# Attention and two mixtures of experts on one core: the projections of the middle stage regrouped, three of them moved to the end of the period ahead, and a new order of all steps

## The chip, the cores and the metric

One NeuronCore of a Trainium2 chip runs the whole program. The metric is the device time of one execution in microseconds (us), lower is better; the number compared is the median over runs.

## The reference

Three layers follow each other on a batch of B = 4 sequences of S = 576 positions, D = 512 columns, all in float32.

```python
# 1: attention, 8 heads of 64: heads 0-3 see the last 32 positions, heads 4-7 every 4th of the last 128
scores = where(mask, (q @ k.T) / 8, -1e9);  x = softmax(scores) @ v            # (B, S, 8*64)
# 2: mixture of 4 causal attention experts, the 2 best of each position
for e in range(4):
    q, k, v = x @ wq[e], x @ wk[e], x @ wv[e]                                  # (B, S, 64)
    ye = softmax(where(causal, -1e9, (q @ k.T) / 8)) @ v @ wo[e]
    out += (gate weight of e at this position) * ye                             # gate: softmax of the 2 best of x @ w_gate
# 3: mixture of 8 feed-forward experts (512 -> 1024 -> 512), one expert a position
e[s] = argmax(logits[s])  if s == 0 or local_gate[s] < 0.5  else e[s - 1]
y[s] = softmax(logits[s])[e] * (relu(out[s] @ w1[e]) @ w2[e])
```

## The kernel before, in words

**Periods.** The first two layers are pipelined over the batch. There are five periods. In period a, TensorE (PE), VectorE (DVE) and ScalarE (ACT) work on layer 1 of sequence a and, at the same time, on layer 2 of sequence m = a - 1. In the first period there is no layer 2 work (m is None), in the last no layer 1 work (a is None). After the five periods DVE and PE work out the routing of layer 3 (`dve_route`, L1599), and the feed-forward experts run slot by slot. The order of the steps in a period is written out by hand, three times: `pe_period` (L801), `act_period` (L1217) and `dve_period` (L1474). Each engine takes its list strictly in order; semaphores tie them together.

**Layer 1 in a period.** Sixteen steps `pe_use` 0 to 15 (L601) transpose queries and keys that the DMAs brought into `raw`, four steps for each of four pairs of heads, through the one PSUM bank `X`; `move_use_d` and `move_use_a` (L1064, L1074) copy them to `qT` and `kT`. Then come 14 groups G of three blocks: `pe_scores` (L620), `dve_mask` (L1371), `act_exp` (L1187), `dve_norm` (L1389), `pe_probs` (L639, the transposes of the probabilities), `move_probs` (L1084), `pe_values` (L652), and `move_x_d`/`move_x_a` (L1107, L1116), which write the result to `XT` or, for the first two pairs of heads, to `xa`. GpSimd (POOL) copies `xa` into `XT` once the projections of the sequence before are done. `pe_values` of group G + 1 waits for the moves of group G, since there is one bank for it.

**Layer 2 in a period.** Thirteen projections `pe_project` 0 to 12 (L673): 0 to 4 are the values with the gate logits (one 128-row tile each, the last 64 rows), 5 to 12 the queries and keys. They go in turn to the two banks `S2`, and `move_proj` (L1137) empties them, even ones on DVE, odd ones on ACT. `dve_gates` (L1401, four parts, with `act_gates` on ACT between) turns the gate logits into `gate`. Then ten units w = 0 to 9: `pe_scores2` (L699), `dve_mask2` and `act_exp2` for each of two heads, `dve_sums2`, `dve_norm2` (which reads `gate`), `pe_probs2` (L724, two halves), `move_probs2`, `pe_values2` (L737), `move_out2`. Two units make one tile of `pe_out` (L755), whose result `move_y` copies out of bank `X` and SP stores. `pe_logits` (L767) makes the router logits of layer 3, `dve_logits` copies them.

**Where a period has nothing to do.** With m None or a None, some steps are skipped and some are replaced by `turn_over` (L615): two products of the identity with itself that nobody reads. `pe_project` and `pe_scores2` do that in the first period, `pe_scores` from group 6 and `pe_values` from group 5 in the last.

**The DMA queue of SP** takes in order, in each period: `load_qk` (L301) of pairs 2 and 3, `load_v` (L312) and the loads for the next period, and `store_y` 0 to 4 (L338); each waits for the step that frees its buffer. Weights, and queries and keys of pair 2 of the first sequence, are issued before the first period.

The period's order on PE before begins and ends so:

```python
pe_project(pe, m, 0); pe_project(pe, m, 1); pe_use(pe, m, a, 0, 0); pe_project(pe, m, 2); ...
... pe_probs2(pe, m, 8, 1); pe_values2(pe, m, 8); pe_probs2(pe, m, 9, 0); pe_probs2(pe, m, 9, 1)
pe_values2(pe, m, 9); pe_logits(pe, m, a); pe_out(pe, m, a, 4, 16)
```

Of the kernel before, what the change touches and what calls it, by code (L numbers as in the profile page):

```python
# [16 lines left out]
P = 128  # L17
# [27 lines left out]
NT = len(TILE)  # L45
# [26 lines left out]
def build(nc, q, k, v, w_gate, wq, wk, wv, wo, w_gate2, w_local, w1, w2, out, xs):  # L72
    with ExitStack() as ctx:
# [276 lines left out]
        def _(sp):  # L350
# [16 lines left out]
            for a in range(B + 1):  # L367
# [304 lines left out]

        def pe_project(pe, m, n):  # L673
            if m is None:
                turn_over(pe, S2[0], 2)
                return
            kind, x, half = proj_piece(n)
            if n == 0:
# [3 lines left out]
                pe.wait_ge(w_loaded, W_LOADS)  # L682
                pe.wait_ge(wor_m, 4)
                if m > 0:
                    pe.wait_ge(masked2, m * SUBS)
            if n >= 2:
                pe.wait_ge(proj_moved[n % 2], m * NPROJ_B[n % 2] + n // 2)
            for c in range(NC):
                if kind == "v":
                    for r in range(0, P, TILE[x]):  # L690
                        last = pe.matmul(S2[n % 2][r:r + TILE[x], 0:VW], XT[:, c, T0[x]:T0[x] + TILE[x]],  # L691
                                         wv_sb[:, c, :], start=(c == 0), stop=(c == NC - 1))
                else:
                    w = wq_sb if kind == "q" else wk_sb
                    last = pe.matmul(S2[n % 2][:, 0:PCOLS], w[:, c, x * P:(x + 1) * P],  # L695
# [3 lines left out]
        def pe_scores2(pe, m, w):  # L699
# [24 lines left out]
        def pe_probs2(pe, m, w, h):  # L724
# [4 lines left out]
            pe.wait_ge(normed2, m * SUBS + c + 1)  # L729
            if m * 2 * UNITS + 2 * w + h > 0:  # L730
# [6 lines left out]
        def pe_values2(pe, m, w):  # L737
# [3 lines left out]
            nq = TILE[t]  # L741
            pe.wait_ge(pt2_moved, m * 2 * UNITS + 2 * w + 2)
# [58 lines left out]
        def pe_period(pe, m, a):  # L801

            pe_project(pe, m, 0)
            pe_project(pe, m, 1)
            pe_use(pe, m, a, 0, 0)
            pe_project(pe, m, 2)
            pe_use(pe, m, a, 1, 0)
            pe_project(pe, m, 3)
            pe_use(pe, m, a, 2, 0)
            pe_project(pe, m, 4)  # L810
            pe_use(pe, m, a, 3, 0)
            pe_project(pe, m, 5)
            pe_scores(pe, a, 0)
            pe_use(pe, m, a, 4, 0)
            pe_project(pe, m, 6)
            pe_scores(pe, a, 1)
            pe_router_turn(pe, m)
            pe_use(pe, m, a, 5, 0)
            pe_probs(pe, a, 0)
            pe_project(pe, m, 7)  # L820
            pe_values(pe, a, 0)
            pe_use(pe, m, a, 6, 0)
            pe_scores(pe, a, 2)
            pe_probs(pe, a, 1)
            pe_project(pe, m, 8)
            pe_use(pe, m, a, 7, 0)
            pe_values(pe, a, 1)
            pe_project(pe, m, 9)
            pe_scores(pe, a, 3)
            pe_probs(pe, a, 2)  # L830
            pe_use(pe, m, a, 8, 0)
            pe_project(pe, m, 10)
            pe_values(pe, a, 2)
            pe_router(pe, m)
            pe_use(pe, m, a, 9, 0)
            pe_scores(pe, a, 4)
            pe_probs(pe, a, 3)
            pe_project(pe, m, 11)
            pe_use(pe, m, a, 10, 0)
            pe_values(pe, a, 3)  # L840
            pe_scores(pe, a, 5)
            pe_probs(pe, a, 4)
            pe_project(pe, m, 12)
            pe_use(pe, m, a, 11, 0)
            pe_values(pe, a, 4)
            pe_scores2(pe, m, 0)
            pe_scores(pe, a, 6)
            pe_probs(pe, a, 5)
            pe_use(pe, m, a, 12, 0)
            pe_scores2(pe, m, 1)  # L850
            pe_values(pe, a, 5)
            pe_scores(pe, a, 7)
            pe_use(pe, m, a, 13, 0)
            pe_probs2(pe, m, 0, 0)
            pe_probs2(pe, m, 0, 1)
            pe_probs(pe, a, 6)
            pe_scores2(pe, m, 2)
            pe_values2(pe, m, 0)
            pe_use(pe, m, a, 14, 0)
# [965 lines left out]
```

## Time and profile before

| | us |
|---|---|
| median of 3 runs (844.21 to 846.16) | 845.7 |
| the profiled execution's own time | 846.1 |
| its span, first to last instruction | 844.4 |
| PE busy | 772.6 (91%) |
| DVE busy | 322.3 (38%) |
| ACT busy | 266.5 (32%) |
| mean granted TensorE clock | 0.952 of full speed |

The five periods fill the span from 0 to 445.4 us; the routing and the feed-forward experts the rest. Busy time of PE counts a matmul for as long as it takes, also where the granted clock is at half, so an idle time and a slow clock have to be looked for separately.

### The profile page before, as it was taken

What the parts mean: (1) busy time and instruction counts of PE and PEld (TensorE: products, weight loads), DVE (VectorE), ACT (ScalarE), POOL (GpSimd) and SP (SyncE); (2) the same over time, 40 slices, a digit from 0 to 9 for tenths busy, and PEclk for the clock granted to TensorE, in tenths of its full rate; (3) what the DMA queues carried; (4) which work ended last, traced back from release to release, by engine and by line L of the source; (5) the groups of instructions that cost most, each with busy time, mean ns of one, the idle gap of its engine ahead of it and who ended that gap; (6) DMA issues with size and microseconds to landing.
All of it is one profiled execution on the core that took longest, in us unless ns stands there. A gap on an engine that the chain in (4) does not pass through costs nothing. (4 is left out here: it accounts for less than half of the span.)

```text
span 844.4 us, 12479 instructions
## 1 busy us (share of the span) xinstructions
PE 772.6 (91%) x3835; PEld 490.0 (58%) x3836; DVE 322.3 (38%) x976; ACT 266.5 (32%) x864; POOL 82.5 (10%) x141
## 2 busy tenths in 40 slices
PE   8879989899989999899987999999999999999980
PEld 8767866578656876576553544545445454444540
DVE  3663587256861588323525611112111121121110
ACT  2662677247761578402430020111101111011000
POOL 4110010000100000000001111101001011010111
PEclk8998999899997999889986999999999999999996
DMA  6852253113620222000003211551151551010010
GB/s 148 167 148 71 56 142 98 39 32 78 177 60 16 58 69 101 26 7 1 28 24 125 98 45 39 224 218 37 37 212 50 223 225 38 25 50 19 26 49 7
DMA packets 88815, 69.62 MB, mean 82 GB/s; under 512 B 78334, under 2 KB 78366, under 8 KB 86848
## 3 DMA queue, kind: packets, MB, share of 16 engines
q1 hardware_dynamic: 81120, 44.73, 18.5%
q0 software_dynamic: 7648, 24.29, 8.7%
q8 instruction: 26, 0.43, 0.2%
q14 instruction: 21, 0.17, 0.1%
HBM read 118.12 MB, written 11.27 MB: 153 GB/s over the span
## 5 line engine op out<-in xcount | busy, mean ns | idle before, releaser
L988 PE MATMUL bank<-w_sb,pt 128*128 x352 | 158.4, 593 | 1.3 <-DVE pt L1765 1.3
L1008 PE MATMUL bank<-w_all,raw_all 128*128 x352 | 154.8, 592 | 2.3 <-DVE raw_all L1769 2.3
L1353 ACT ACTIVATE raw_all<-bank 128x512 f32<-128x512 f32 x44 | 26.3, 597 | 270.3 <-PE bank L988 270.3
L1008 PEld LDWEIGHTS bank<-w_all,raw_all 128*128 128x128 f32 x352 | 65.4, 191 | 76.2 <-issue 76.2
L988 PEld LDWEIGHTS bank<-w_sb,pt 128*128 128x128 f32 x352 | 64.0, 192 | 65.2 <-issue 65.2
L1778 DVE TENSOR_SCALAR raw_all<-bank,p_slot 128x512 f32 x22 | 16.5, 751 | 156.6 <-PE bank L1008 149.4
L695 PE MATMUL bank<-stage_b,w_all 128*128 128x288 f32 x256 | 66.9, 409 | 0.0
L1196 ACT ACTIVATE pr<-sm,negmax_a 96x80 f32<-96x80 f32 (+1 forms) x168 | 59.7, 358 | 8.8 <-DVE negmax_a L1387 8.6
L570 POOL DMA_INDIRECT out_dram<-raw_all,idx x25 | 25.4, 1017 | 288.9 <-DVE raw_all L1778 274.5
L695 PEld LDWEIGHTS bank<-stage_b,w_all 128*128 128x128 f32 x256 | 46.7, 190 | 11.2 <-issue 0.4
L1185 ACT COPY w_sb<-bank 128x256 f32<-128x256 f32 (+3 forms) x81 | 34.6, 427 | 44.5 <-PE bank L733 43.9
L1769 DVE COPY raw_all<-bank 128x512 f32<-128x512 f32 x44 | 30.2, 686 | 46.7 <-PE bank L997 46.7
L1765 DVE COPY pt<-bank 128x512 f32<-128x512 f32 x23 | 15.9, 692 | 82.4 <-PE bank L974 82.4
L763 PE MATMUL bank<-w_all,OT 128*128 128x512 f32 (+1 forms) x80 | 45.5, 697 | 0.0
L635 PE MATMUL bank<-kT,qT 128*96 128x80 f32 (+1 forms) x336 | 43.5, 267 | 1.9 <-DVE negmax_a L1387 1.1
L733 PE MATMUL bank<-ident,heads_out 128*128 128x128 f32 (+1 forms) x200 | 37.0, 283 | 9.0 <-ACT w_sb L1185 8.4
L751 PE MATMUL bank<-w_sb,V 128*64 128x128 f32 (+2 forms) x480 | 33.3, 273 | 11.5 <-ACT w_sb L1185 11.3
L635 PEld LDWEIGHTS bank<-kT,qT 128*96 128x96 f32 (+1 forms) x336 | 38.8, 181 | 5.8 <-DVE negmax_a L1387 2.3
L691 PE MATMUL bank<-w_all,stage_b 128*128 128x260 f32 (+1 forms) x192 | 40.4, 402 | 0.5 <-DVE stage_b L1114 0.5
L733 PEld LDWEIGHTS bank<-ident,heads_out 128*128 128x128 f32 (+1 forms) x200 | 22.8, 142 | 30.2 <-issue 23.0
L997 PEld LDWEIGHTS bank<-ident,raw_all 128*128 128x128 f32 x176 | 27.8, 204 | 19.8 <-issue 19.8
L751 PEld LDWEIGHTS bank<-w_sb,V 128*64 128x64 f32 (+1 forms) x480 | 23.7, 143 | 21.5 <-ACT w_sb L1185 19.5
(212 smaller groups left out, 1029.6 us busy)
## 6 DMA issues: line engine op xcount, KB each, us to landing
w_sb<-in_moe_w_dram SPq DMA_DIRECT2D x19, 2048.0 KB
w_all<-in_moe_w_dram SPq DMA_DIRECT2D x19, 2048.0 KB
w_sb<-in_moe_w_dram POOLq DMA_DIRECT2D x12, 512.0 KB, 4.2
w_all<-in_moe_w_dram POOLq DMA_DIRECT2D x12, 512.0 KB, 4.1
raw_all<-in_q_dram SPq DMA_DIRECT2D x32, 144.0 KB
raw_all<-in_k_dram SPq DMA_DIRECT2D x32, 144.0 KB
mixture_rows<-y_sb SPq DMA_DIRECT2D x16, 256.0 KB, 2.0
v_dil<-in_v_dram SPq DMA_DIRECT2D x48, 80.0 KB, 2.6
```

What stands on the lines that cost most here:

```text
L635: last = pe.matmul(SA[0:M, m * nk:(m + 1) * nk], qT[s][:, blk * M:(blk + 1) * M], kT[s][:, k0:k0 + nk], start=True, stop=True)
L691: last = pe.matmul(S2[n % 2][r:r + TILE[x], 0:VW], XT[:, c, T0[x]:T0[x] + TILE[x]], wv_sb[:, c, :], start=(c == 0), stop=(c == NC - 1))
L695: last = pe.matmul(S2[n % 2][:, 0:PCOLS], w[:, c, x * P:(x + 1) * P], XT[:, c, half * PCOLS:(half + 1) * PCOLS], start=(c == 0), stop=(c = ...
L733: last = pe.transpose(PT[0:TILE[kb], n * P:(n + 1) * P], pr2[c % 2][:, T0[kb]:T0[kb] + TILE[kb]], ident[:, :])
L751: last = pe.matmul(O2[h * DH:(h + 1) * DH, 0:nq], V[0:nk, kb, e * DH:(e + 1) * DH], ptm[0:nk, w % 2, c0:c0 + nq], start=(kb == 0), stop=(k ...
L763: last = pe.matmul(X[0:nq, :], OT[:, p, T0[t]:T0[t] + nq], wo_sb[:, p, :], start=(p == 0), stop=(p == PAIR_E - 1))
L988: last = pe.matmul(ps[half], xT[:, c * P:(c + 1) * P], w1_sb[:, bass.ds(buf, 1), c * F + half * HALF:c * F + (half + 1) * HALF].rearrange( ...
L997: last = pe.transpose(ps[2 + half][:, c * P:(c + 1) * P], hid[:, half * HALF:(half + 1) * HALF].rearrange("x (m c) -> x c m", c=4)[:, c, : ...
L1008: last = pe.matmul(ps[5], hidT[:, n * P:(n + 1) * P], w2_sb[:, bass.ds(buf, 1), n // 4, (n % 4) * D:(n % 4 + 1) * D].rearrange("p o n -> p ...
L1185: return nc.scalar.copy(o, i)
L1196: last = nc.scalar.activation(pr4[G % 4][0:M, m * nk:(m + 1) * nk], sm4[G % 4][0:M, m * nk:(m + 1) * nk], ACT.Exp, bias=negmax[G % 4][0:M, ...
L1769: nc.vector.tensor_copy(hidT[:, half * HALF:(half + 1) * HALF], ps[2 + half]).then_inc(hT_moved[half], 1)
```

## The change: what it does

Five things. (1) The pieces are renumbered: 0 to 7 are now queries and keys, 8 to 12 values with gate logits. (2) The value pieces go to the banks `PT` and `O2` (those of `pe_probs2` and `pe_values2`), by the new `proj_bank`, so `S2` is free for `pe_scores2` once the eight others are moved; its wait is cut to those, and the waits for the rest go to `pe_probs2`, `pe_values2` and `dve_gates`. (3) `pe_project(pe, a, 0)`, `1` and `2` stand at the end of the period ahead, behind the layer 1 work of the sequence that they project. (4) `pe_logits` comes after `pe_out` of tile 4, no longer before it. (5) All three lists are in a new order; SP stores y of tile 3 before it loads the values of pair 1. With m None, `turn_over` runs for pieces 3 to 12 only; with a None the three at the end are `turn_over`s into `SA`.

```diff
                 if m >= 0:
                     store_y(sp, m, 2)
+                if m >= 0:
+                    store_y(sp, m, 3)
                 if a + 1 < B:
                     load_v(sp, a + 1, 1)
                 if m >= 0:
-                    store_y(sp, m, 3)
                     store_y(sp, m, 4)
...
-            if n < NT:
-                return "v", n, 0
-            r = n - NT
-            return ("q", "k")[r % 2], (r // 2) % 2, r // 4
+            if n < 8:
+                return ("q", "k")[n % 2], (n // 2) % 2, n // 4
+            return "v", n - 8, 0
...
+        def proj_bank(n):
+            return S2[n % 2] if n < 8 else (PT, O2)[n % 2]
...
         def pe_project(pe, m, n):
             if m is None:
-                turn_over(pe, S2[0], 2)
+                turn_over(pe, S2[0] if n >= 3 else SA, 2)
                 return
...
                 pe.wait_ge(w_loaded, W_LOADS)
+                if m > 0:
+                    pe.wait_ge(masked2, m * SUBS)
+            if n == 8:
                 pe.wait_ge(wor_m, 4)
                 if m > 0:
-                    pe.wait_ge(masked2, m * SUBS)
-            if n >= 2:
+                    pe.wait_ge(pt2_moved, m * 2 * UNITS)
+                    for p in range(PAIR_E):
+                        pe.wait_ge(o2_moved[p], m * NT)
+            elif n >= 2 and n != 9:
                 pe.wait_ge(proj_moved[n % 2], m * NPROJ_B[n % 2] + n // 2)
+            to = proj_bank(n)
...
             if w == 0:
                 for half in range(2):
-                    pe.wait_ge(proj_moved[half], (m + 1) * NPROJ_B[half])
+                    pe.wait_ge(proj_moved[half], m * NPROJ_B[half] + 4)
...
             pe.wait_ge(normed2, m * SUBS + c + 1)
+            if w == 0 and h == 0:
+                pe.wait_ge(proj_moved[0], (m + 1) * NPROJ_B[0])
...
+            if w == 0:
+                for half in range(2):
+                    pe.wait_ge(proj_moved[half], (m + 1) * NPROJ_B[half])
             pe.wait_ge(pt2_moved, m * 2 * UNITS + 2 * w + 2)
...
             if part == 0:
                 dve.wait_ge(stage_b_ready, 1)
-                dve.wait_ge(proj_moved[0], m * NPROJ_B[0] + 3)
-                dve.wait_ge(proj_moved[1], m * NPROJ_B[1] + 2)
+                for half in range(2):
+                    dve.wait_ge(proj_moved[half], (m + 1) * NPROJ_B[half])
```

The new order on PE, written short (U `pe_use`, J `pe_project`, S P V `pe_scores`, `pe_probs`, `pe_values` of a group; s p v the same of layer 2, with unit and half; Y `pe_out`; R the two router steps, first period only):

```
U0 J3 U1 J4 U2 J5 U3 J6 U4 S0 J7 U5 S1 R J8 U6 S2 s0 U7 J9 P0 U8 S3 s1 U9 J10 S4 V0 U10 J11 S5 J12
P1 U11 P2 V1 S6 s2 P3 U12 p0.0 V2 R p0.1 S7 v0 p1.0 P4 p1.1 V3 U13 S8 s3 v1 p2.0 P5 V4 p2.1 U14 s4 S9
U15 P6 v2 p3.0 V5 S10 p3.1 Y0 V6 P7 S11 s5 P8 p4.0 V7 v3 p4.1 S12 s6 P9 p5.0 v4 V8 p5.1 s7 Y1 p6.0 S13
P10 v5 V9 p6.1 s8 P11 Y2 p7.0 V10 v6 p7.1 P12 V11 s9 P13 p8.0 v7 V12 p8.1 Y3 p9.0 V13 v8 p9.1
J0 of the next sequence, v9, J1 of the next, Y4, logits, J2 of the next
```

On DVE the four parts of `dve_gates` stand behind `move_proj` 12 and ahead of `dve_sums2` of unit 0 and the first `dve_norm2`. On ACT `act_gates` stands behind `move_probs` of group 1 and ahead of `move_use_a` 11 and `move_probs` 2.

## Rows read from the trace of the kernel before

**Rows 1.** The page: busy time of PE, and its granted clock in 40 slices.
```profile
PE 772.6 (91%) x3835; PEld 490.0 (58%) x3836; DVE 322.3 (38%) x976; ACT 266.5 (32%) x864; POOL 82.5 (10%) x141
...
PEclk8998999899997999889986999999999999999996
```
**Rows 2.** Busy time by stretch: five periods, then the rest; us, engines, PEclk, DMA share, GB/s.
```profile
0.00:66.80 66.80, 54.45 (x422) 50.12 (x424) 34.10 (x101) 33.88 (x128) 17.10 (x64) 0.93 0.69 154
66.80:166.60 99.80, 92.48 (x636) 68.98 (x636) 57.64 (x199) 55.77 (x198) 3.43 (x6) 0.94 0.31 80
166.60:265.40 98.80, 91.48 (x637) 68.48 (x636) 58.32 (x200) 55.70 (x198) 3.43 (x6) 0.95 0.30 77
265.40:364.20 98.80, 91.48 (x637) 68.54 (x636) 58.32 (x200) 55.70 (x198) 3.43 (x6) 0.95 0.20 56
364.20:445.40 81.20, 73.45 (x431) 50.13 (x430) 29.33 (x106) 24.69 (x74) 0.18 (x1) 0.94 0.04 15
445.40:844.40 399.00, 369.23 (x1075) 183.74 (x1075) 84.57 (x171) 40.81 (x68) 54.96 (x59) 0.96 0.26 93
```
**Rows 3.** Whom PE waited for in the third period: us in total, times, longest.
```profile
PE bank L751 <- ACT w_sb L1185: 2.7, 5, 0.7
PE bank L733 <- ACT w_sb L1185: 2.0, 3, 0.8
PE bank L648 <- DVE pr L1398: 1.5, 2, 0.9
```
**Rows 4.** Busy time by stretch: within a period, then around the ends of periods.
```profile
107.00:149.00 42.00, 38.38 (x292) 26.84 (x290) 33.56 (x123) 32.53 (x121) 2.76 (x5) 1.00 0.45 121
149.90:159.60 9.70, 6.87 (x74) 4.47 (x74) 2.94 (x10) 4.15 (x10) 0.00 (x0) 1.00 0.29 78
159.60:166.70 7.10, 7.10 (x23) 4.25 (x22) 0.21 (x1) 0.00 (x0) 0.00 (x0) 0.52 0.01 2
257.50:265.40 7.90, 7.90 (x24) 5.03 (x24) 0.21 (x1) 0.00 (x0) 0.00 (x0) 0.50 0.00 0
356.30:364.30 8.00, 8.00 (x25) 5.12 (x25) 0.20 (x1) 0.00 (x0) 0.00 (x0) 0.50 0.01 2
```
**Rows 5.** PE in order of time: start, us, line, form, count.
```profile
66.81 5.80 PE L691 MATMUL bank<-w_all,stage_b 128*128 128x260 f32 x16 [0.54 <-DVE stage_b L1114]
...
152.04 1.96 PE L763 MATMUL bank<-w_all,OT 128*128 128x512 f32 x4
...
159.22 3.94 PE L778 MATMUL bank<-wor,OT 128*128 128x9 f32 x20 [0.37 <-issue]
163.09 3.64 PE L763 MATMUL bank<-w_all,OT 128*64 128x512 f32 x4
166.66 3.77 PE L691 MATMUL bank<-w_all,stage_b 128*128 128x260 f32 x16
...
176.94 2.15 PE L695 MATMUL bank<-stage_b,w_all 128*128 128x288 f32 x8
```
**Rows 6.** Weight loads of `pe_logits` (L778): ns least, median, most, over the run.
```profile
L778 PEld LDWEIGHTS bank<-wor,OT x80: 186/333/338, 159.2 to 440.6; 128*128 128x128 f32 x80
```
**Rows 7.** DVE in order of time: the first and last of thirteen steps of `dve_gates`.
```profile
177.28 0.17 DVE L1412 TENSOR_REDUCE g<-V 128x5 f32<-128x20 f32 x1
...
180.01 0.36 DVE L1435 COPY gate_z<-gate 64x2 f32<-64x2 f32 x2
```
**Rows 8.** First period: a wait of PE, one `turn_over`, `pe_use` 12 on PE.
```profile
PE bank L648 <- DVE pr L1398: 4.7, 8, 0.8
...
25.68 0.61 PE L618 MATMUL bank<-ident 128*128 128x128 f32 x4
...
39.01 0.42 PE L611 MATMUL bank<-ident,raw_all 72*128 72x72 f32 x4
```
**Rows 9.** SP's queue: the last loads that `pe_use` 12 needs.
```profile
29.76 1.63 SPq L309 DMA_DIRECT2D raw_all<-in_k_dram  x2
```
**Rows 10.** Start of the routing, PE and DVE in order of time.
```profile
445.41 7.61 PE L940 MATMUL bank<-causal,ident 128*128 128x512 f32 x12 [0.78 <-DVE y_sb L1362]
...
447.62 0.18 DVE L1649 SCALAR_TENSOR_TENSOR kv<-r,r 128x20 f32<-128x20 f32 x1
```

More of the change, by code:

```diff
@@ L813, in pe_period @@
+            pe_use(pe, m, a, 4, 0)
             pe_scores(pe, a, 0)
-            pe_use(pe, m, a, 4, 0)
-            pe_project(pe, m, 6)
+            pe_project(pe, m, 7)
+            pe_use(pe, m, a, 5, 0)
             pe_scores(pe, a, 1)
             pe_router_turn(pe, m)
[L818 to L821, printed above, removed]
+            pe_project(pe, m, 8)
             pe_use(pe, m, a, 6, 0)
             pe_scores(pe, a, 2)
+            pe_scores2(pe, m, 0)
@@ L824, in pe_period @@
+            pe_use(pe, m, a, 7, 0)
+            pe_project(pe, m, 9)
+            pe_probs(pe, a, 0)
+            pe_use(pe, m, a, 8, 0)
+            pe_scores(pe, a, 3)
+            pe_scores2(pe, m, 1)
+            pe_use(pe, m, a, 9, 0)
+            pe_project(pe, m, 10)
+            pe_scores(pe, a, 4)
+            pe_values(pe, a, 0)
+            pe_use(pe, m, a, 10, 0)
+            pe_project(pe, m, 11)
+            pe_scores(pe, a, 5)
+            pe_project(pe, m, 12)
             pe_probs(pe, a, 1)
-            pe_project(pe, m, 8)
@@ L826, in pe_period @@
-            pe_use(pe, m, a, 7, 0)
+            pe_use(pe, m, a, 11, 0)
+            pe_probs(pe, a, 2)
             pe_values(pe, a, 1)
[L828 to L832, printed above, removed]
+            pe_scores(pe, a, 6)
+            pe_scores2(pe, m, 2)
+            pe_probs(pe, a, 3)
+            pe_use(pe, m, a, 12, 0)
+            pe_probs2(pe, m, 0, 0)
             pe_values(pe, a, 2)
@@ L849, in pe_period @@
[L849 to L852, printed above, removed]
-            pe_use(pe, m, a, 13, 0)
[L854 to L859, printed above, removed]
-            pe_values(pe, a, 6)
+            pe_probs2(pe, m, 0, 1)
+            pe_scores(pe, a, 7)
+            pe_values2(pe, m, 0)
@@ new lines, in pe_period @@
+            pe_probs(pe, a, 5)
+            pe_values(pe, a, 4)
+            pe_probs2(pe, m, 2, 1)
+            pe_use(pe, m, a, 14, 0)
+            pe_scores2(pe, m, 4)
+            pe_scores(pe, a, 9)
+            pe_use(pe, m, a, 15, 0)
+            pe_probs(pe, a, 6)
+            pe_values2(pe, m, 2)
+            pe_probs2(pe, m, 3, 0)
+            pe_values(pe, a, 5)
+            pe_scores(pe, a, 10)
+            pe_probs2(pe, m, 3, 1)
+            pe_out(pe, m, a, 0, 16)
+            pe_values(pe, a, 6)
@@ new lines, in pe_period @@
+            pe_probs(pe, a, 7)
+            pe_scores(pe, a, 11)
+            pe_scores2(pe, m, 5)
+            pe_probs(pe, a, 8)
+            pe_probs2(pe, m, 4, 0)
+            pe_values(pe, a, 7)
+            pe_values2(pe, m, 3)
+            pe_probs2(pe, m, 4, 1)
+            pe_scores(pe, a, 12)
+            pe_scores2(pe, m, 6)
+            pe_probs(pe, a, 9)
+            pe_probs2(pe, m, 5, 0)
+            pe_values2(pe, m, 4)
+            pe_values(pe, a, 8)
+            pe_probs2(pe, m, 5, 1)
@@ L885, in pe_period @@
+            pe_scores2(pe, m, 7)
             pe_out(pe, m, a, 1, 16)
+            pe_probs2(pe, m, 6, 0)
+            pe_scores(pe, a, 13)
+            pe_probs(pe, a, 10)
+            pe_values2(pe, m, 5)
             pe_values(pe, a, 9)
-            pe_probs2(pe, m, 4, 0)
-            pe_probs(pe, a, 10)
-            pe_scores2(pe, m, 6)
-            pe_probs2(pe, m, 4, 1)
+            pe_probs2(pe, m, 6, 1)
+            pe_scores2(pe, m, 8)
+            pe_probs(pe, a, 11)
+            pe_out(pe, m, a, 2, 16)
```

430 lines of the change are left out of this document (196 added, 234 removed).

## The prediction, made before the changed kernel was run

> **What bounds the kernel now.** I first read the page: PE is busy 91% of the span, and no other engine over 38% [rows 1]. So the question is what PE's time is made of. The second view, busy time by stretch, splits it: the reader should see that the feed-forward stage, 399.0 us, holds nothing that the diff touches, and that in each full period (98.8 us) PE is busy 91.5, while DVE and ACT have under 59 us of work each [rows 2]. The five periods, 445.4 us, are PE's in-order list, with two kinds of loss in it.
>
> The first is **idle time**: 98.8 - 91.48 = 7.3 us in each full period, 81.2 - 73.45 = 7.75 in the last, 66.8 - 54.45 = 12.35 in the first [rows 2]. The view of waits says what ends it: `pe_values2` and `pe_probs2` wait 0.4 to 0.9 us at a time for an ACT copy, `pe_probs` for a DVE scaling [rows 3]. These are links of one chain (transpose, copy, product) with too little other work on PE between them.
>
> The second is **the clock**. The page's digits dip at intervals of about a period [rows 1]; the stretches show why: from 149.9 to 159.6 PE is busy only 6.87 of 9.7 us, in small transposes and products, at clock 1.00; then it runs 7.1 us without any idle time at 0.52, the 1.2 GHz level, and returns to 2.4 GHz in the projections that follow. The next two ends spend 7.9 and 8.0 us at 0.50 [rows 4]. An output product of four matmuls takes 1.96 us at the full clock and 3.64 in the dip; a pair of value projections 3.77 against 5.80 (the latter behind the first period) [rows 5]. PE's busy time hides this.
>
> The Trainium skill ("TensorE: Matmul & The Clock Gate", section "Why this matters for your kernels") says that a throughput drop in mid-kernel is avoided by leaving no long idle gap between bursts of matmuls. Here the clock fell behind gaps of at most 0.9 us each [rows 3, 4], so the trace disagrees with the rule taken alone. By it, what I add to the tail would be worth nothing to the clock; that is rival B below.
>
> **The change, part by part.** The sum is made on the profiled execution, 846.1 us (span 844.4 and 1.7 around it), which lies 0.4 above the median of 845.7, inside the spread of the three runs.
>
> *Three projections in the tail.* Projection 0 now stands between `pe_probs2` 9.1 and `pe_values2` 9, projection 1 between that and the output product, projection 2 behind the logits. Each is 8 matmuls, some 2.0 us on PE (2.15 with the overlap of the next, [rows 5]), longer than the copies that `pe_values2` and `pe_out` wait for (waits of at most 0.8, [rows 3]). PE's idle 9.7 - 6.87 = 2.8 us of each tail [rows 4] falls to about 0.3. No work is added: the same thirteen projections run. What the first projection must wait for is `move_x` of group 13, queued on DVE and ACT behind a few short steps; between `pe_values` 13 and the projection stand one `pe_values2` and one `pe_probs2`, about 1.2 us, against a copy of some 0.5. I charge nothing; without that cover it costs 0.5, as in the 0.54 of [rows 5].
>
> *The clock.* The stretch ahead of the logits then holds dense wide matmuls in place of 71% busy. I expect no fall at the three inner boundaries. Worth: output product 3.64 - 1.96 = 1.7 [rows 5]; logits 3.94 us, which are bound by weight loads of 333 ns in the dip against 186 at best [rows 6], so 3.94 x 186/333 = 2.2 and a gain of 1.7; together 3.4. At the second and third boundary the dip is 0.8 and 0.9 us longer [rows 4] and reaches into `pe_values2` and the projection, worth 0.4 and 0.5 more. Sum 3.4 + 3.8 + 3.9 = 11.1. Lower end 0 (it still falls), upper end 11.1 plus the 2.0 at 66.8 us, which I leave in place, since the tail of the first period has no layer 2 work.
>
> *Idle time in the body of a period.* Softmax of layer 2 now starts behind eight projections, not thirteen, and scores run further ahead of probabilities (P3 behind S6, where before P3 stood behind S4). I walked the new list by hand with the durations of this period. `pe_probs` no longer waits for DVE: 1.5 us off [rows 3]. But new waits come between J12 and Y0, where ACT and DVE have a full queue: the gates are now on the chain. `move_proj` 12 (0.45), thirteen gate steps from 177.28 to 180.37 = 3.1 us [rows 7], then sums, one move and a scaling, some 1.0, must pass before `pe_probs2` 0.0; PE has 3.5 us of other work for these 4.6, so it waits 1.1. ACT's gate exponential waits for the first two gate steps with `move_use_a` 11 and `move_probs` 2 queued behind it: P2 and P3 wait up to 0.4. Eight more waits of 0.2 to 0.5 up to V5 make 2.5. I end at about 4.5 us idle a period in place of 7.3: 3 x 2.8 = 8.4 saved. Ends: 0 (waits only move) and 3 x 6.
>
> *First period.* Three `turn_over`s fewer, 0.5 each [rows 8]: 1.5. Of the 12.35 idle [rows 2], 4.7 are `pe_probs` waiting for DVE [rows 8], which the deeper order removes; against it, `pe_values` 12 and 13 and projection 0 now follow with little between, at 0.5 each, and the `pe_use` steps come earlier than their data. `pe_use` 12 ran at 39.01 [rows 8]; the last load that it needs is issued until 29.76 + 1.63 = 31.4 [rows 9] and SP, not a wait, sets that. With some 3 us to land it can't run before 34.5, so at most 4.5 us come off up to there. Behind it I count 22 us of PE work and 3.5 of waits, which ends at 60, against 66.8: 6.7 saved. Ends 3 and 10.
>
> *Last period.* No layer 1 work covers the gates: behind J12 PE has one `turn_over` and `pe_scores2` 2, 1.1 us, for 4.6 (with no move of x, 4.2), so it waits 3.1, of which 0.8 is paid back by units 0 and 1, scored earlier, and 0.6 by the wait for the last projection that falls away: 1.5 lost net. The three tail `turn_over`s (1.5) fill about as much idle time. The clock there stays as it was.
>
> *Logits last.* DVE may start the routing right behind the logits' copy, 0.5 us sooner than behind the 0.68 us copy of y. DVE's own lead buys nothing: it is done at 447.8 and waits until 452.9 for PE's filler products, 7.61 us in the dip [rows 10]. 0.5 saved.
>
> *SP and banks.* `store_y` 3 ahead of `load_v` of pair 1: that load is used by V3 of the next period, over 30 us later. `PT` and `O2` are empty when pieces 8 and 9 come. Both zero.
>
> Sum: 11.1 + 8.4 + 6.7 - 1.5 + 0.5 = 25.2, and 846.1 - 25.2 = 820.9; I say **821**.
>
> **The rivals.** *B, the clock still falls at the inner ends:* the logits are nine columns wide and remain, and the tail still ends in 64-column products. 821 + 11.1 = **832**. For it: the fall needed no long gap. Against: everything from J0 on is dense. *C, the waits only move:* ACT and DVE are in order, and between J12 and Y0 their queues are full, where before layer 2 came later. Idle stays 7.3, and the first period gains only 3: 821 + 8.4 + 3.7 = **833**. *D, both:* the three-part gain is gone, **844**, which is no change or just outside. *E, slower: the dip moves to the middle.* From J12 to Y0 the list now has transposes of one to three blocks with waits between, much like the tail of before (71% busy, then 0.52) [rows 4]. The Trainium skill (same page, section "Part 4: PE-mode transpose") says that transposes don't count as activity in the same way. From 107 to 149 us transposes were frequent too, with PE at 91% busy, and the clock was 1.00 [rows 4], so the trace bears it out only in part. If the clock fell at J12 and stayed down to Y0, some 17 us of PE work would take 1.7 times as long (between 5.80/3.77 = 1.5 and 3.64/1.96 = 1.9, [rows 5]): 12 us in each of three periods, 821 + 36 = **857**. It decides from 12 us of work at the low clock in each period (12 x 0.7 = 8.4, a third of the gain).
>
> **How the numbers follow.** The forecast 0.55, B 0.14, C 0.14, D 0.06, E 0.06, and 0.05 for a gain over 836 left as a mixture of B and C. The range must leave out at most 0.2: it runs from 811 (idle down by 6 a period would give 811, at the upper bound of that term) to 837, which takes in B, C and their mixture. A measurement of this kernel can tell about 0.2%, 1.7 us, from no change. Faster by more: 0.55 + 0.14 + 0.14 + 0.05 = 0.88. D splits into 0.04 the same and 0.02 slower; with E slower is 0.08.
>
> **What would show it.** Right: the first projection starts near 60 us, the next ones (projection 0) come 91 to 93 us apart, the clock's digits have no dip at the three inner ends, `pe_logits` takes about 2.2 us there, and `pe_probs2` waits for DVE (the scaling at L1464) once a period by about 1 us, 3 in the last. Wrong: a granted clock near 0.5 in the tail (B) or between J12 and Y0 (E); PE's idle time at 7 or more in a full period (C); a wait of `pe_use` 8 or 12 for its DMA over 2 us; or routing that starts later than 422.

## The result, and the profile after

Four runs of after have a median of **818.63 us** (816.3 to 823.13), beside 845.93 for the kernel before: a ratio of 0.9692, 95% interval 0.9663 to 0.9721. Another six runs of the same kernel, beside the first experiments, gave 818.26 (810.33 to 824.61), 0.9657 [0.9607, 0.9706]. Forecast were 821, and faster with 0.88. Medians and ranges here and below are of all runs of a kernel; the ratios leave out the runs more than 1.5% above its fastest.

The page of after, to be held against [rows 1]: as many matmuls, 8.7 us less of busy time in them, and low digits of the clock in other places: 8 and 7 from 184 to 225 us, and 6 from 368 to 388 us.

```profile
PE 763.9 (93%) x3835; PEld 488.7 (60%) x3836; DVE 324.2 (40%) x992; ACT 262.1 (32%) x848; POOL 82.3 (10%) x141
...
PEclk9888999998799999996998999999999999999996
```

Busy time by stretch of after, cut at the starts of the first projections of each period, as [rows 2] (length, then PE, PEld, DVE, ACT, POOL, the granted clock, DMA share, GB/s):

```profile
0.00:61.40 61.40, 50.56 (x410) 48.33 (x411) 33.87 (x101) 34.07 (x128) 16.35 (x63) 0.91 0.71 153
61.40:148.20 86.80, 84.25 (x592) 64.69 (x593) 57.72 (x201) 53.57 (x192) 3.97 (x7) 0.97 0.36 94
148.20:244.20 96.00, 94.20 (x638) 71.55 (x637) 58.82 (x204) 54.57 (x195) 3.43 (x6) 0.91 0.31 80
244.20:333.30 89.10, 86.62 (x638) 66.02 (x637) 58.53 (x204) 54.51 (x195) 3.43 (x6) 1.00 0.25 67
333.30:417.80 84.50, 79.38 (x488) 54.81 (x486) 30.46 (x112) 24.56 (x73) 0.54 (x1) 0.92 0.06 21
417.80:817.30 399.50, 368.86 (x1076) 183.27 (x1075) 84.76 (x171) 40.81 (x68) 54.57 (x58) 0.96 0.25 92
```

The feed-forward stage took 399.5 us against 399.0, so all 27.1 us of difference between the two spans are in the periods. The cuts of after lie ahead of `v9`, `Y4` and the logits, which no longer belong to the period in front of the cut, some 5.0 us; with that shifted back, the first period gave 5.3 us, the three inner ones 297.4 - 276.9 = 20.5, the last 81.2 - 79.5 = 1.7, and the route lost 0.5. A full period without any dip of the clock is the one from 244.2: 89.10 us for 98.8.

PE in order of time at the first inner end, where [rows 5] has the dip (start, us, line, form, count): the logits take 2.40 us instead of 3.94, in the full clock, behind `Y4` and ahead of projection 2.

```profile
153.27 1.93 PE L777 MATMUL bank<-w_all,OT 128*64 128x512 f32 x4
155.13 2.40 PE L792 MATMUL bank<-wor,OT 128*128 128x9 f32 x20
157.39 2.19 PE L704 MATMUL bank<-stage_b,w_all 128*128 128x288 f32 x8
```

The stretches around that end, and then the two places where the clock fell in this execution, each behind the stretch that leads to it:

```profile
142.00:148.20 6.20, 6.20 (x63) 4.63 (x62) 2.51 (x8) 3.36 (x9) 0.00 (x0) 1.00 0.11 42
148.20:157.40 9.20, 9.20 (x63) 6.27 (x61) 1.27 (x3) 1.33 (x4) 0.00 (x0) 1.00 0.35 90
...
187.00:197.00 10.00, 8.20 (x69) 6.57 (x68) 8.93 (x39) 7.28 (x29) 0.67 (x1) 1.00 0.18 40
197.00:214.50 17.50, 17.50 (x76) 12.76 (x77) 10.02 (x37) 10.82 (x43) 0.00 (x0) 0.51 0.17 39
...
365.00:369.10 4.10, 0.86 (x7) 0.34 (x6) 3.48 (x19) 0.22 (x1) 0.00 (x0) 0.84 0.00 0
369.10:382.00 12.90, 11.31 (x48) 6.73 (x49) 5.89 (x26) 4.81 (x19) 0.00 (x0) 0.52 0.00 1
```

From 142.0 to 157.4 PE has no idle time at all, against 2.8 us in the tail of before [rows 4], and the clock stays at 1.00. The dip from 197.0 to 214.5 is 17.5 us of busy PE at 1.2 GHz, and it is the whole difference between the second full period (96.0) and the third (89.1). The last lies behind the wait for the gates.

Whom PE waited for in the period from 244.3 to 333.4, all five lines (line, for whom, us in total, times, longest): 2.4 us in place of the 7.3 idle of before.

```profile
PE bank L744 <- DVE heads_out L1478: 0.7, 1, 0.7
PE bank L648 <- ACT pt L1106: 0.7, 2, 0.4
PE bank L765 <- ACT w_sb L1199: 0.5, 1, 0.5
PE bank L635 <- DVE negmax_a L1401: 0.3, 1, 0.3
PE bank L744 <- ACT w_sb L1199: 0.2, 1, 0.2
```

### The profile page after: what moved, and what is told of

It reads as the page before. It is cut to its first block and busy times, and to the rows that moved or that the text cites. A ratio compares the mean times of both kernels' runs of the same rounds, so it can differ in the third digit from the quotient of the medians.

```text
span 817.3 us, 12480 instructions
## 1 busy us (share of the span) xinstructions
PE 763.9 (93%) x3835; PEld 488.7 (60%) x3836; DVE 324.2 (40%) x992; ACT 262.1 (32%) x848; POOL 82.3 (10%) x141
## 5 line engine op out<-in xcount | busy, mean ns | idle before, releaser
L1022 PE MATMUL bank<-w_all,raw_all 128*128 x352 | 156.5, 598 | 2.2 <-DVE raw_all L1783 2.2
L704 PE MATMUL bank<-stage_b,w_all 128*128 128x288 f32 x256 | 70.4, 425 | 0.5 <-DVE stage_b L1128 0.5
L704 PEld LDWEIGHTS bank<-stage_b,w_all 128*128 128x128 f32 x256 | 48.6, 198 | 12.8 <-DVE stage_b L1128 0.8
L570 POOL DMA_INDIRECT out_dram<-raw_all,idx x25 | 25.4, 1017 | 291.6 <-DVE raw_all L1792 275.7
L744 PE MATMUL bank<-ident,heads_out 128*128 128x128 f32 (+1 forms) x200 | 38.9, 294 | 7.8 <-DVE heads_out L1478 5.7
L777 PE MATMUL bank<-w_all,OT 128*128 128x512 f32 (+1 forms) x80 | 39.7, 621 | 0.0
L618 PE MATMUL bank<-ident 128*128 128x128 f32 x192 | 33.7, 314 | 1.6 <-POOLq L446 1.6
```

The costliest lines, as they stand in the source:

```text
L618: pe.matmul(to[:, 0:P], ident[:, :], ident[:, :], start=True, stop=True)
L704: last = pe.matmul(to[:, 0:PCOLS], w[:, c, x * P:(x + 1) * P], XT[:, c, half * PCOLS:(half + 1) * PCOLS], start=(c == 0), stop=(c == NC - 1))
L744: last = pe.transpose(PT[0:TILE[kb], n * P:(n + 1) * P], pr2[c % 2][:, T0[kb]:T0[kb] + TILE[kb]], ident[:, :])
L777: last = pe.matmul(X[0:nq, :], OT[:, p, T0[t]:T0[t] + nq], wo_sb[:, p, :], start=(p == 0), stop=(p == PAIR_E - 1))
L1022: last = pe.matmul(ps[5], hidT[:, n * P:(n + 1) * P], w2_sb[:, bass.ds(buf, 1), n // 4, (n % 4) * D:(n % 4 + 1) * D].rearrange("p o n -> p ...
```

## The experiments

Two theories stood against each other. Mine, the forecast's: three projections in the tail and the logits last keep the clock up at the ends, and the order of the body shortens waits. The rival: the new order of the body does nearly all of it, and what is put at the end hardly matters. A third question came up on the way, what a short wait costs. Edits are against the kernel after unless said otherwise; ratios are to the kernel before.

**The same kernel again.** No edit.

> The changed kernel, unchanged, to see its spread. My theory: its inner period ends keep the full clock, but the stretch between J12 and Y0 may fall to the low clock in any of three periods, each time for about 7 us (period of 96.0 against 89.1 us), so runs lie near 816, 819 or 823 rather than within 2 us of each other. Rival: the 7 us between 816.3 and 823.1 are noise of another kind, and the three full periods of this trace differ by under 2 us.

Six runs: 810.33, 812.09, 815.73, 820.78, 821.72 and 824.61 us, with mean granted clocks of 0.965, 0.963, 0.957, 0.948, 0.947 and 0.943. The order of the times is the order of the clocks. In the profiled one, 810.33, the periods took 58.3, 85.6, 89.1, 90.8 and 85.0 us, and none of them has the dip of the 96.0; the last period's is there as before. So the mid-period dip does not come in every execution. What varies from run to run is how often the clock falls, not the work.

The 90.8 has a short fall of another kind, right behind the logits of the second inner end (239.99 to 242.4), with PE busy without a gap since 200 us:

```profile
233.00:243.20 10.20, 10.20 (x66) 7.11 (x65) 1.27 (x3) 1.39 (x4) 0.00 (x0) 1.00 0.34 87
243.20:246.80 3.60, 3.60 (x13) 2.56 (x12) 0.93 (x3) 0.39 (x1) 0.00 (x0) 0.53 0.00 0
```

Projections 2 and 3 take 3.13 and 2.69 us there, for the 2.19 and 2.15 of the end before it.

**Projections at the head of their own period.** The body's order is kept.

```diff
+            pe_project(pe, m, 0)
+            pe_project(pe, m, 1)
+            pe_project(pe, m, 2)
             pe_use(pe, m, a, 0, 0)
...
-            pe_project(pe, a, 0)
             pe_values2(pe, m, 9)
-            pe_project(pe, a, 1)
             pe_out(pe, m, a, 4, 16)
             pe_logits(pe, m, a)
-            pe_project(pe, a, 2)
```

> Projections 0 to 2 go back to the head of their own period; all else as in the changed kernel. Theory (the tail projections keep the clock up and cover the chain there): the low clock returns at the inner period ends, 11 us over three of them, and idle time of about 2 us comes back in each: 818.6 + 11 + 6 = 835. Rival (the new order of the rest does it all): no dip at the ends, 819 to 822.

Measured 822.78 us (821.93 to 826.09), 0.973 [0.9696, 0.9765]. Its inner end, and the full period behind it, by stretch; then its logits:

```profile
149.00:158.30 9.30, 8.46 (x79) 5.82 (x78) 1.48 (x4) 1.97 (x5) 0.00 (x0) 1.00 0.25 68
158.20:249.80 91.60, 88.28 (x638) 67.25 (x639) 58.76 (x204) 54.49 (x194) 3.44 (x6) 0.98 0.33 84
```
```profile
155.90 2.40 PE L792 MATMUL bank<-wor,OT 128*128 128x9 f32 x20
```

Without a single projection in the tail PE is busy 8.46 of 9.3 us there, and the logits run at the full clock all the same. But behind them the clock falls, at this end and at the third, and the three projections that follow here take 7.76 us, where they take 6.07 at the second end, which has no fall. The stretch of the fall, and then one in the first period, right behind the router step:

```profile
159.30:162.80 3.50, 3.50 (x9) 2.49 (x8) 0.46 (x1) 0.00 (x0) 0.00 (x0) 0.51 0.14 41
36.40:53.20 16.80, 16.80 (x90) 16.75 (x91) 8.87 (x27) 10.21 (x42) 1.23 (x2) 0.50 0.29 65
```

The move of three projections is worth 4.5 us of the 27, with intervals that overlap at their ends, and not all of it is won at the ends of periods. It takes 0.8 us of idle time out of each. The first period of this run, which has its three `turn_over`s back and these 16.8 us at the low clock, took 66.1 us, for 61.4 and 58.3 in the two profiled runs of after. The rival was right on the logits, and nearly right on the time.

**The same, and the logits ahead of Y4.** Now the end is in the old order altogether.

```diff
-            pe_out(pe, m, a, 4, 16)
             pe_logits(pe, m, a)
+            pe_out(pe, m, a, 4, 16)
```

> As e1, and pe_logits ahead of pe_out of tile 4 as well, so that only the new order of the rest is left of the change. Theory (in e1 the clock at the inner ends held because the output product and the logits then follow units that are less starved; the logits in front bring the old tail back): logits take near 4 us at the inner ends again and the time is 830 to 835. Rival (the new body alone keeps the clock, wherever logits and projections stand): logits at 2.4 us, and the time is within 2 us of e1, 821 to 825.

Measured 825.24 us (819.76 to 831.6, four runs), 0.9744 [0.9683, 0.9806]. By stretch at the same end, then PE in order:

```profile
150.60:160.20 9.60, 8.84 (x92) 6.31 (x90) 3.88 (x12) 5.36 (x14) 0.00 (x0) 1.00 0.07 28
...
162.60:165.90 3.30, 3.30 (x5) 0.72 (x4) 0.00 (x0) 0.00 (x0) 0.00 (x0) 0.50 0.47 104
```
```profile
160.27 2.37 PE L792 MATMUL bank<-wor,OT 128*128 128x9 f32 x20 [0.38 <-issue]
162.57 3.60 PE L777 MATMUL bank<-w_all,OT 128*64 128x512 f32 x4
```

Tail like before's, logits like before's, yet the clock holds through the logits and falls only at `Y4`: what ran into it was 92% busy (8.84 of 9.60), where before it was 71% [rows 4]. It falls so at all three inner ends (`Y4` takes 3.60, 3.20 and 2.65 us), and this run has a dip of 16 us in the middle of its first full period besides (112.0 to 128.2, clock 0.50). The order of the body alone gives some 20 of the 27 us (16 to 27 by the interval). The logits' place is worth 2.5 us between the medians, inside both intervals.

**Keys loaded ahead of values.** PE's longest wait in the first period of after is `pe_use` 8, for a DMA: 3.56 us at 23.78. SP's order is changed.

```diff
-            load_v(sp, 0, 1)
             load_qk(sp, 0, 2)
+            load_v(sp, 0, 1)
```

> SP issues the queries and keys of pair 2 of the first sequence ahead of the values of pair 1; all else as in the changed kernel. Theory: the 3.6 us wait of pe_use 8 in the first period goes, and the low clock behind it (24 to 30 us) too: the first projection starts at 57 in place of 61.5, and the time falls by 4 to 5 us to 814. Rival: pe_use 12, whose loads SP issues no sooner than before, catches what is gained, and the time falls by under 1 us.

A miss: 824.52 us (821.4 to 826.56), 0.9733 [0.9696, 0.977], some 6 slower than after. That wait is gone, but `pe_use` 12 then waits 4.50 us for its own load, which stands behind thirteen weight loads on SP's queue. The clock falls inside that wait, at 32.6, and stays low until 59.8, though PE has no idle time once the wait is over:

```profile
34.37 0.71 PE L611 MATMUL bank<-ident,raw_all 72*128 72x72 f32 x4 [4.50 <-DMA raw_all<-in_k_dram]
```
```profile
34.40:59.80 25.40, 25.40 (x132) 25.32 (x133) 10.53 (x32) 11.87 (x48) 1.89 (x3) 0.50 0.31 75
```

The first projection came at 72.2 us, not 61.5. The wait that grew did so by about a microsecond over the one removed (4.50 for 3.56); ten were lost up to there, with the clock down for 27 us. Behind the first projection this run lost nothing: its full periods took 86.1, 89.2 and 90.8 us.

**Filler where PE waits for the gates.** Identity products into empty banks, which add work and remove none: two products ahead of `pe_probs2` 0.0 (fourteen in the last period) and two ahead of `pe_values2` 1.

```diff
+            pe_fill(pe, m, a, 0)
             pe_probs2(pe, m, 0, 0)
...
+            pe_fill(pe, m, a, 1)
             pe_values2(pe, m, 1)
```

> The changed kernel with products of the identity that nobody reads at two waits of the middle: one pair ahead of pe_probs2 0.0 (seven pairs in the last period) and one ahead of pe_values2 1, into the banks that these write next. Nothing is taken off. Theory (low activity between J12 and Y0 lets the clock fall): no low clock after pe_probs2 0.0 in any period, the last period 4 to 5 us shorter, 810 to 814 in the median and runs closer together. Rival (the clock there falls for another reason, or the filler only adds its 1 us a period): 818 to 822.

Measured 816.75 us (810.55 to 819.85), 0.9646 [0.9601, 0.9691]: not told apart from after by its time. The stretches tell more, the last period and then a mid-period:

```profile
336.20:417.40 81.20, 78.92 (x521) 56.13 (x520) 30.59 (x112) 24.47 (x73) 0.54 (x1) 1.00 0.07 22
196.00:212.00 16.00, 15.72 (x80) 12.37 (x80) 9.51 (x36) 9.86 (x39) 0.51 (x1) 0.55 0.25 58
```

The last period has the full clock throughout and is 3.3 us shorter than after's 84.5 with more work in it. The dip in the middle of a full period came all the same, so filling these two places does not keep it away; this part stayed inconclusive.

**The old order with three projections in the tail.** Edits against the kernel before: pieces renumbered, projections 0 to 2 in the tail and logits last as in after, the gates behind projection 12; all else in the old order.

```diff
-            pe_project(pe, m, 0)
-            pe_project(pe, m, 1)
             pe_use(pe, m, a, 0, 0)
-            pe_project(pe, m, 2)
...
+            pe_project(pe, a, 0)
             pe_values2(pe, m, 9)
-            pe_logits(pe, m, a)
+            pe_project(pe, a, 1)
             pe_out(pe, m, a, 4, 16)
+            pe_logits(pe, m, a)
+            pe_project(pe, a, 2)
```

> The kernel of before with only the renumbering, the three projections (queries and keys) in the tail, the logits behind Y4, and the gates behind J12; banks and order of the rest as before. Theory (about half of the gain is the tail's, half the new order's): clock kept at the inner ends, 11 us, tail idle 2 us each, less 1 to 3 us in each period for the gates now on the chain: 832 to 836. Rival (the tail alone does nearly all of it, as the forecast had 11 + 3 x 2.5 for it): 826 to 829. Rival the other way (gates behind J12 in the old order cost more than the tail gives): 840 or more.

The surprise of the study: 867.76 us (866.75 to 872.23), 1.0268 [1.0231, 1.0305], slower than the kernel that it was to improve. A wait in the middle of a period, what follows it, and the whole period:

```profile
212.07 0.70 PE L647 MATMUL bank<-ident,pr 96*80 96x96 f32 x3 [2.40 <-DVE pr L1397]
```
```profile
212.00:230.00 18.00, 17.30 (x84) 13.77 (x85) 11.04 (x47) 10.82 (x44) 1.70 (x3) 0.50 0.35 84
165.40:269.30 103.90, 96.02 (x638) 72.06 (x637) 59.06 (x204) 55.03 (x194) 3.44 (x6) 0.90 0.29 73
```

The first inner end holds the full clock from projection 0 to the logits, as forecast for this step. At the second it falls right behind the logits, for 3 us; at the third at projection 0, which takes 3.87 us for 2.18. The first end, and the fall at the second:

```profile
165.40:175.00 9.60, 9.60 (x63) 6.61 (x62) 1.27 (x3) 0.77 (x2) 0.00 (x0) 1.00 0.06 14
279.00:282.00 3.00, 3.00 (x10) 1.99 (x9) 0.00 (x0) 0.00 (x0) 0.00 (x0) 0.54 0.00 0
```

And a dip of 18 us stands in the middle of a period: PE waits 2.40 us for a scaling that is queued on DVE behind the gates, then is 96% busy at the low clock. This is rival E's mechanism, in the old order.

**The same with the gates early.** I took the one wait for the cause and moved it away: pieces 4 to 8 are the values, the gates follow in four parts between DVE's earlier steps.

```diff
-            if n < 8:
-                return ("q", "k")[n % 2], (n // 2) % 2, n // 4
-            return "v", n - 8, 0
+            if 4 <= n < 9:
+                return "v", n - 4, 0
+            r = n if n < 4 else n - 5
+            return ("q", "k")[r % 2], (r // 2) % 2, r // 4
```

> As e5 (old order, three projections in the tail, logits last), but with the values as pieces 4 to 8 and the gate steps spread over DVE ahead of unit 0, as in e6. Theory (e5 lost by one wait of 2.4 us behind the gates, which let the clock fall for 20 us in each period; the tail itself is worth its 11 us and more): no low clock in the body, 826 to 832, faster than before by 14 to 20 us. Rival (the projections in the tail themselves hurt the old order, say by the layer 1 chain being uncovered at the head of the period): over 840 even so.

Measured 860.01 us (857.39 to 865.77), 1.0207 [1.0161, 1.0253]. My theory fell: the 2.40 us wait is gone, PE idles 7.8 us in that period, half a microsecond more than in one of before, and the dip is there. A shorter wait leads to it, with 4 us at 61% busy around it:

```profile
213.21 0.49 PE L712 MATMUL bank<-stage_b 64*128 64x128 f32 x4 [1.40 <-DVE negmax L1447]
```
```profile
212.00:216.00 4.00, 2.45 (x21) 2.21 (x21) 3.46 (x17) 2.92 (x13) 0.00 (x0) 0.94 0.50 114
216.00:232.00 16.00, 15.28 (x63) 10.58 (x62) 10.17 (x40) 7.93 (x32) 1.71 (x3) 0.50 0.50 132
```

So it is not that wait. The theory that remained: a cluster of short waits between small transposes can let the clock fall, and then costs many times itself.

**The same with filler.** A test of it by added work alone, in full and last periods, against the kernel just above.

```diff
+        def pe_fill(pe, m, to, n):
+            if m is not None:
+                turn_over(pe, to, n)
...
+            pe_fill(pe, m, PT, 6)
             pe_scores2(pe, m, 1)
...
+            pe_fill(pe, m, O2, 2)
             pe_probs2(pe, m, 0, 1)
```

> As e5b (old order, tail projections, gates early, 860), with identity products nobody reads at its two starved places: three pairs ahead of pe_scores2 1, where PE waits 1.4 us and the next 17 us run at the low clock, and one pair ahead of pe_probs2 0.1. Work is only added. Theory (rival E's mechanism: it is the clock that falls behind those waits which makes e5b slow): the low stretch of 17 us goes in each full period, some 8 us each: 834 to 840. Rival (PE is simply short of work there and the clock is a companion): the filler costs its 1 to 2 us a period and the time stays at 857 or more.

Measured 839.38 us (838.39 to 841.14, eight runs), 0.9919 [0.9887, 0.9951]: 20.6 us less, by products that nobody reads. The filler and the same instruction behind it; then the 7 us around it, the 16 that follow (they answer to the two stretches above), and the whole period:

```profile
204.79 1.28 PE L618 MATMUL bank<-ident 128*128 128x128 f32 x10
...
206.10 0.49 PE L716 MATMUL bank<-stage_b 64*128 64x128 f32 x4
```
```profile
202.00:209.00 7.00, 6.64 (x64) 6.07 (x63) 5.58 (x26) 5.10 (x21) 0.67 (x1) 1.00 0.37 84
209.00:225.00 16.00, 14.14 (x103) 9.48 (x102) 14.12 (x53) 12.08 (x49) 1.69 (x3) 1.00 0.62 149
...
157.30:255.80 98.50, 91.34 (x654) 68.40 (x653) 57.93 (x200) 55.63 (x198) 3.43 (x6) 0.98 0.31 78
```

The period is 98.5 us, where it was 104.6, and PE still idles 7.2 of them, as in the kernel before (98.8 and 7.3, [rows 2]), even with 1.86 us without work in the 16 of the second row. Over the period the idle time hardly changed (7.8 to 7.2 us); the low clock behind it went. The three full periods gave 6.3, 6.1 and 4.9 us, 17.3 of the 17.9 between the two spans. Short falls of some 3 us are left at two of the three ends. And the kernel after is 21 us faster still than this old order whose clock holds.

**Gates before the last projections.** Again in the kernel after: the first halves of queries and keys, then values and gate logits, then the second halves, so that the gates are done long before projection 12.

```diff
-            if n < 8:
-                return ("q", "k")[n % 2], (n // 2) % 2, n // 4
-            return "v", n - 8, 0
+            if 4 <= n < 9:
+                return "v", n - 4, 0
+            r = n if n < 4 else n - 5
+            return ("q", "k")[r % 2], (r // 2) % 2, r // 4
...
+            dve_gates(dve, m, 0)
             dve_mask(dve, a, 3)
```

> The values with the gate logits become pieces 4 to 8 and the second halves of queries and keys 9 to 12, all in the banks PT and O2, and the gate steps are spread ahead of unit 0 on DVE; positions in the lists as in the changed kernel. Theory (the gates were put on the chain behind J12): the 3.2 us wait in the last period and 0.7 in each full one go, and with them most low-clock stretches in the middle: 5 to 12 us less, 807 to 814. Rival (the middle waits for ACT and DVE throughput, not for the gates): under 3 us less, since the wait only moves to the next copy.

Measured 809.76 us (801.83 to 816.71), 0.9543 [0.9495, 0.959]. PE's wait for the gates is gone, and the last period falls from 84.5 to 81.3 us:

```profile
326.70:408.00 81.30, 78.69 (x488) 54.76 (x486) 29.29 (x107) 25.27 (x77) 0.54 (x1) 0.94 0.06 20
```

The full periods took 82.9, 88.2 and 89.8 us, against after's 86.8, 96.0 and 89.1 (85.6, 89.1 and 90.8 in its other profiled run). The first period of the profiled run was a bad one, 65.8 us, with the low clock from 38 to 55 us, behind the router step.

**And the loads early.** To that, all of sequence 0's keys and queries are loaded ahead of the weights of layer 2, which cures what the loads experiment ran into.

```diff
-            load_v(sp, 0, 1)
             load_qk(sp, 0, 2)
+            load_v(sp, 0, 1)
+            load_qk(sp, 0, 3)
```

> As e6, and SP issues queries and keys of pairs 2 and 3 of the first sequence ahead of the layer 2 weights (pair 2 also ahead of the values of pair 1). Theory (in e3 the wait only moved from pe_use 8 to pe_use 12, whose loads stood behind 13 weight loads): both waits go, the first projection starts at 54 to 57 with the clock up, and the time is 798 to 803. Rival (the first period's clock falls anyway, its work being small): first projection at 60 or later, 806 to 810 as e6.

Measured 804.84 us (801.83 to 808.05), 0.9508 [0.9473, 0.9544]. The DMA waits of the first period are gone and the first projection is at 60.25, yet the clock is still low from 33.8 to 47 us, right behind the router's nine-column products, and from 56 to 64. Once more beside the last kernel:

> e8 unchanged, as the measure for e9 on the same chip: 802 to 808, median near 805.

803.51 us (800.11 to 804.54), 0.9512 [0.9475, 0.955].

**Filler in the first and the last period.** Two identity products at each of six waits there, the full periods untouched.

```diff
+        def pe_fill_first(pe, m):
+            if m is None:
+                turn_over(pe, S2[0], 2)
...
             pe_router(pe, m)
+            pe_fill_first(pe, m)
...
+            pe_fill_first(pe, m)
             pe_values(pe, a, 11)
```

> e8 with pairs of identity products nobody reads at waits: in the first period behind the router step and ahead of V11, V13 and the first projection, in the last ahead of pe_probs2 0.0 and pe_values2 1. Theory (what is left over is low clock in those two periods: 32 to 47 us, 56 to 64 and 356 to 370): most of it goes, 5 to 9 us less than e8, 796 to 800. Rival (as e4, the clock falls in other places by chance and the filler costs its own 0.5 us each): within 2 us of e8.

Measured 800.59 us (793.86 to 806.3), 0.9507 [0.946, 0.9553], the lowest of all, though 2.9 under the kernel without filler, with intervals that lie in each other, is not a difference shown. Behind the router step the clock stays at 1.00 in this run, where it is low for some 13 us in both profiled runs without the filler; but in after's two it stays up with no filler too, so one run does not show that the filler did it. The profiled run is the fastest seen, 793.86; by stretch, first and last period:

```profile
0.00:56.50 56.50, 50.74 (x426) 48.77 (x427) 33.48 (x101) 34.28 (x128) 16.42 (x63) 0.94 0.77 162
317.60:395.00 77.40, 75.10 (x493) 52.78 (x491) 28.98 (x106) 25.33 (x77) 0.54 (x1) 1.00 0.06 21
```

## Why the prediction was right, and where it was not

The total was right, 821 against 818.6, and the likeliest case was the one that came. Its terms, held against after:

- *The clock at the ends, 11.1.* It happened in this execution: no dip at any of the three inner ends, logits at 2.40 us (I had said 2.2), an output product at 1.93 instead of 3.64. **But the reason I gave is the weak step**: "the stretch ahead of the logits then holds dense wide matmuls". For the logits it was not needed: with none in the tail they ran at the full clock too, 2.40 and 2.37 us, behind a tail whose idle time the new body order had taken from 2.8 us to 0.8. Nor is dense work enough: in eight profiled runs of kernels with the new body and these three projections in the tail, the clock fell right behind the logits at 6 of 24 inner ends, for some 3 us, with PE busy throughout. Without them it did so at 5 of 6. So by these few counts the move makes the fall rarer, and where it comes behind logits that stand last it costs 1.5 to 1.7 us, not the 3.4 to 3.9 that I had priced. Between the medians, what stands in the tail is worth 4.5 us here, a good part of it in the first period, 7 with the logits' place. In the old order the move, together with the renumbering and the later gates, lost 14 to 22, as the dip came back in the body. I had added up parts whose worth hangs on each other.
- *Idle time in the body, 8.4.* Undersold: 2.5, 1.8 and 2.5 us idle in the full periods, and not 4.5; a saving of 5 a period in place of 2.8. The wait for the gates was forecast at 1.1 and measured 0.7, the others 1.8 where I had 3.4.
- *What I left at zero: a fall of the clock in the body.* It was rival E, at 12 us in each of three periods and a chance of 0.06. It came once, 17.5 us long, in one of three periods, and cost 96.0 - 89.1 = 6.9 us. Over the three inner periods gains and this loss made 20.5, beside 19.5 forecast: two errors of the same size, in opposite directions, so that it came so near is luck. That runs of after lie between 810 and 825 us in the order of their clocks fits a fall that comes in some executions and not in others.
- *First period, 6.7.* It gave 5.3. `pe_use` 8 waited 3.56 us for its load, which I had named as a sign of being wrong, "a wait of `pe_use` 8 or 12 for its DMA over 2 us". I had walked the load of `pe_use` 12 only, which was right: not before 34.5, and it ran at 35.00. The clock was low from 24 to 30 us and from 56 to 64 (0.51 and 0.57).
- *Last period, a loss of 1.5, with 0.5 back for the logits.* The wait for the gates came as worked out, 3.24 us for 3.1. Not priced was what follows it, 12.9 us at 0.52 (369.1 to 382.0, above); against that, the low clock at the end of the last period, which I had left in place, was gone. The last 9 to 10 us ahead of the routing, before and then after:

```profile
436.00:445.40 9.40, 8.26 (x28) 5.20 (x28) 1.15 (x4) 0.00 (x0) 0.18 (x1) 0.51 0.00 0
```
```profile
408.00:417.80 9.80, 9.79 (x88) 7.00 (x86) 1.21 (x4) 1.55 (x4) 0.54 (x1) 1.00 0.16 51
```

Net the period gained 1.7 us. The 0.5 for the logits did not show: the stage behind took 0.5 us more than before, although the filler products at its start took 5.39 us for the 7.61 of [rows 10]; where that went is open. Without the wait it has 3.2 more to give, as two experiments showed.
- *SP and banks, zero.* None of PE's waits in the third full period is for a transfer or a bank's copy out of a projection; right.

Rival B, the clock still falling at the inner ends, was wrong for the first profiled run of after; it came true in small, behind the logits, at one end of the second, and at five of six with no projections in the tail. The Trainium skill's rule of long idle gaps ("TensorE: Matmul & The Clock Gate", section "Why this matters for your kernels") fits the three waits of 3.24, 3.56 and 4.50 us, inside each of which the clock fell. It does not cover the rest: the longest gap ahead of the dip in the old order with early gates was 1.40 us, in 4 us that were 61% busy, and behind the logits of the second run of after it fell with no gap at all.

Still open: why the mid-period dip of after comes in some executions and not in others. The stretch ahead of it was 82% busy (8.20 of 10.0 us) in the run that had it; one period on, the same products with nearly the same waits were busy 8.27 of 10.0, and the clock held:

```profile
283.10:293.10 10.00, 8.27 (x70) 6.63 (x68) 8.99 (x39) 7.43 (x29) 0.67 (x1) 1.00 0.19 44
```

Filler at two places did not stop it. It stands in 3 of 18 full periods of the new body with the gates late (six profiled runs), and in none of 12 with the gates early (four), too few to tell. Open too is why the clock falls behind the logits or the router step in some runs only.

## What to carry to other kernels

Where the clock can fall, a short wait has two prices: its own length, and some 6 to 7 us if it stands in a cluster that lets the clock go (6.9 in a period of after, 5.8 on average in each of the three of the old order); look at the granted clock of the stretch behind a wait before pricing it at its length. A list for an in-order engine is to be judged as a whole: moving three projections to the tail was worth 4.5 us in one order and, with the renumbering and the later gates that came with it, lost 14 in another, so test the part in both orders. Idle time that can't be removed can be filled, with a few identity products into an empty bank (20.6 us in the old order; at two places of the new one, nothing that the time could tell), and a long chain such as the gates is best started from inputs that are computed first.

## What the runs showed of the hardware that I had not expected

- **The clock falls behind short gaps, and behind nine-column products with no gap, and stays low through busy work.** 2.45 us busy of 4.0 with one wait of 1.40 us, then 16 us at 0.50 while PE was 15.28 of 16 us busy; in after, 17.5 us without any idle time at 0.51; behind the long wait of the loads experiment, 25.4 us at 0.50 without any idle time. Behind the logits it fell in the second profiled run of after with PE busy since 200 us, and behind the router step, which has nine-column products too, in five of the ten profiled runs with the new body, for 13 to 19 us (in a sixth it was low already). The work in these stretches is transposes and small products; in after the stretch ended with an output product, `Y0` (3.22 us at 211.47, 1.88 in the period before it). The Trainium skill (same page, section "Part 4: PE-mode transpose") says that transposes don't count as activity in the same way. That fits here, while the 42 us at 1.00 with frequent transposes [rows 4] show that alone they don't bring the clock down.
- **The spread between runs is the clock's.** Same kernel, 810.33 at a mean of 0.965 and 824.61 at 0.943; the old order with filler, which has no low stretch in its body, had the narrowest spread of the experiments (838.39 to 841.14).
- **Products of nine columns are not cheap.** Twenty of them take 2.40 us at the full clock, 120 ns each, for 3.94 mostly at the low one. Their weight loads last 192 ns in the median of all eighty, where 333 was the median before [rows 6]; twenty in a row would be 3.84 us, so they overlap. That both shrank by nearly the same factor fits a bound by the loads, which is argued and not shown:

```profile
L792 PEld LDWEIGHTS bank<-wor,OT x80: 186/192/193, 155.1 to 417.1; 128*128 128x128 f32 x80
```
